# Attention with V scaled and the decay applied out of PSUM, routing in PSUM, and a new order inside the MoE step

## What is computed

```
# 1. attention with decay: B=4, H=8, S=768, head_dim=64
gamma[h] = 1 - 2 ** (-5 - h)
state = gamma * state + k_t v_t^T              # per head, 64 x 64
y_t   = q_t @ state / sqrt(64)
x = y as 3072 rows (tokens) of 512
# 2. mixture of experts: E=8, F=1024, one expert for each token
e = argmax(x @ w_gate)
x = softmax(x @ w_gate)[e] * sigmoid(x @ w_output_gate)[e] * (relu(x @ w1[e]) @ w2[e])
# 3. feed-forward: 512 -> 2048 -> 512
h = x @ w_in;  out = (h - tanh(h)) @ w_out
```

## Time and profile before

| | |
|---|---|
| time, median of 3 runs | 1131.85 us (1128.59 to 1132.87) |
| the profiled execution: time, span | 1125.78 us, 1124.0 us |
| granted TensorE clock over the span | 0.976 |
| busy: TensorE, VectorE, ACT, POOL | 1047.3, 784.1, 337.6, 382.6 us |
| attention | to about 157 us |
| MoE, with the tables ahead of it | about 157 to 559 us |
| feed-forward | about 559 us to the end |

### The profile page before, as it was taken

How to read it: one execution, slowest core, us unless ns; L and a number is a source line. 1 busy time by engine, 2 the same in 40 slices (tenths; PEclk the granted TensorE clock), 3 DMA queues, 4 the chain that set the end, 5 groups by cost and what they waited for, 6 DMA issues and landing times.

```text
span 1124.0 us, 18489 instructions
## 1 busy us (share of the span) xinstructions
PE 1047.3 (93%) x5577; PEld 866.1 (77%) x5578; DVE 784.1 (70%) x1267; ACT 337.6 (30%) x631; POOL 382.6 (34%) x316
## 2 busy tenths in 40 slices
PE   8988885999999979999679999999999999999998
PEld 7867684787777868878568887887888788788887
DVE  3888977555655556655257777877876877787775
ACT  2432322232322322222013333333333333333333
POOL 2455549665956786791470000000000000000000
PEclk9998998999999999999889999999999999999999
DMA  9976645767767677784320001001001000100101
GB/s 341 330 255 206 229 153 181 230 214 225 238 217 245 206 251 231 220 252 153 135 57 10 20 10 47 19 9 47 9 19 37 19 19 25 31 0 0 38 1 38
DMA packets 78308, 139.56 MB, mean 124 GB/s; under 512 B 7744, under 2 KB 39872, under 8 KB 78272
## 3 DMA queue, kind: packets, MB, share of 16 engines
q1 hardware_dynamic: 31280, 77.73, 21.0%
q10 hardware_dynamic: 43152, 48.77, 13.6%
q0 software_dynamic: 3840, 12.59, 3.4%
HBM read 100.00 MB, written 39.06 MB: 124 GB/s over the span
## 4 chain that ended last, share of the span: by engine, by line
PE 59%; DMA 17%; DVE 13%; issue 6%; ACT 2%; ACTq 1%; POOL 1%; DVEq 0%; SPq 0%; POOLq 0%
PE banks L1104 11%; PE banks L1106 10%; PE banks L1105 10%; DMA hid_quads<-hid_rows 7%; PE banks L1196 7%; PE banks L1198 7%; PE banks L1197 7%; DMA hid_rows<-hid 7%; DVE onehot L691 2%; DVE hidT L854 2%; DMA vn_sb<-in_vn 1%; PE banks L1005 1%; ACT hid L570 1%; PE banks L1012 1%; DVE q_scaled L713 1%
## 5 line engine op out<-in xcount | busy, mean ns | idle before, releaser
L397 POOL TENSOR_TENSOR w_sb<-raw,w_sb 128x1024 fp32r<-128x1024 f32 x80 | 198.3, 2479 | 6.7
L1196 PE MATMUL banks<-x2T_hi,w_sb 128*128 (+1 forms) x384 | 152.9, 398 | 5.2 <-DVE g_sb L947 5.2
L1198 PE MATMUL banks<-x2T_lo,w_sb 128*128 (+1 forms) x384 | 150.4, 392 | 0.0
L1197 PE MATMUL banks<-x2T_hi,w_sb 128*128 (+1 forms) x384 | 150.3, 391 | 0.0
L410 POOL DMA_INDIRECT gathered<-y_sorted,row_back x20 | 22.3, 1117 | 374.4 <-DVE x_sb L912 373.8
L1106 PE MATMUL banks<-w_sb,g_hi 128*128 128x512 f32 x384 | 149.4, 389 | 0.0
L1104 PE MATMUL banks<-w_sb,g_lo 128*128 128x512 f32 x384 | 149.4, 389 | 0.0
L1105 PE MATMUL banks<-w_sb,g_hi 128*128 128x512 f32 x384 | 149.4, 389 | 0.0
L854 DVE STREAM_TRANSPOSE hidT<-hid_quads 128x512 f32<-128x512 f32 x62 | 63.0, 1094 | 115.0 <-DMA hid_quads<-hid_rows 115.0
L1104 PE MATMUL banks<-w_sb,xsT_lo 128*128 (+1 forms) x248 | 101.5, 409 | 28.9 <-DVE xsT_lo L813 26.9
L622 ACT ACTIVATE square<-banks 128x512 f32<-128x512 f32 x96 | 57.4, 597 | 195.0 <-PE banks L1198 195.0
(11 more groups left out here) (135 smaller groups left out, 1890.7 us busy)
## 6 DMA issues: line engine op xcount, KB each, us to landing
raw<-in_weights SPq DMA_DIRECT2D x80, 512.0 KB, 4.0
hid_rows<-hid ACTq DMA_DIRECT2D x31, 512.0 KB, 4.1
hid_quads<-hid_rows ACTq DMA_DIRECT2D x31, 512.0 KB, 4.4
xs_sb<-x_sorted ACTq DMA_DIRECT2D x124, 64.0 KB, 3.0
y_sorted<-ys_sb ACTq DMA_DIRECT2D x31, 256.0 KB, 2.4
kT_sb<-in_kT SPq DMA_DIRECT2D x24, 256.0 KB
qT_sb<-in_qT SPq DMA_DIRECT2D x24, 256.0 KB
kn_sb<-in_kn SPq DMA_DIRECT2D x24, 256.0 KB
```

The source lines that it names most:

```text
L397: nc.gpsimd.tensor_tensor(w_sb[:, s, 1, lo:hi], raw[:, p % RAW_SLOTS], w_sb[:, s, 0, lo:hi].bitcast(fp32), ALU.subtract).then_inc(piece_do ...
L1196: T.matmul(out_, w_lo, hi, start=first, stop=False)
L1197: T.matmul(out_, w_hi, hi, start=False, stop=False)
L1198: return T.matmul(out_, w_hi, lo, start=False, stop=last)
```

## The change

Attention:

- V is scaled in place of K: POOL's `scale_values` multiplies V by the decay of its position, for all 24 tiles, and both `to_state` and `from_chunk` use the scaled V. The mask is then plain causal, one 128x128 table read by broadcast. Q isn't scaled at all: VectorE's `decay_rows` multiplies the sum in bank 3 by q_decay on its way to `xT_sb`. Only bank 3 is used for the sum, so `from_state` of the next tile waits for `decay_rows`.
- The tables of q_decay for chunks 1 to 5 are made by POOL (`make_q_decay`) from the first and a factor for each head; before, they were loaded. Inputs of a tile come in two transfers of 512 KB (keys and queries, then K and V by token). The tables and the zero fill of `x_sorted` are issued on ACT's queue.
- `rows_and_logits` takes the place of router parts, transposes and sum: four products of xT with the identity and the gates side by side, 144 columns each, into banks 5 and 6. ACT copies the rows out; VectorE's `add_logits` reduces over the four parts.
- `logits` and `ranked` lie in PSUM. The routing uses tensor_tensor with a broadcast operand in place of tensor_scalar and scalar_tensor_tensor. The ranks accumulate in one bank over the tiles, from the region's first row up, with an upper and a lower triangular product, so `seen` and the cast go. `find_row` has two instructions instead of four and runs two tiles behind.
- TensorE's order is from_chunk(c), rank(t - 2), scores(c + 1), from_state(c + 1), to_state(c + 1), rows_and_logits(t). `x_sb` has six slots instead of three. POOL waits for the first xsT_lo before it splits set 1.

MoE: a new order in the step, on ACT and on VectorE, and around the last tiles.

```diff
+            def scale_values(t):
...
+                nc.gpsimd.tensor_tensor(v_scaled[:, c % RING].rearrange("p (h d) -> p h d", h=HEADS),
+                                        vn_sb[:, c % RING].rearrange("p (h d) -> p h d", h=HEADS),
+                                        k_decay_sb[:, c].unsqueeze(2).to_broadcast([P, HEADS, HEAD_DIM]),
+                                        ALU.mult).then_inc(v_scaled_done, 1)
...
+            def add_logits(t, last=False):
...
+                V.reduce_sum(one(logits, t), x_parts[:, :, P:X_COLS].rearrange("p k e -> p e k"), AX).then_inc(logits_made, 1)
...
-                V.tensor_scalar(one(onehot, t), ranked[:, 0], route[:, 0:1], None, ALU.is_equal).then_inc(onehot_done, 1)
...
+                V.tensor_tensor(one(onehot, t), ranked[:, 1], route[:].to_broadcast([P, EXPERTS]), ALU.is_equal)\
+                 .then_inc(onehot_done, 1)
...
-                V.tensor_tensor(q_scaled[:, c % 2], qT_sb[:, c % RING], q_decay_sb[:, c], ALU.mult)\
-                 .then_inc(q_scaled_done, 1)
+            def decay_rows(t, c):
+                dve.wait_ge(y_done, t + 1)
+                V.tensor_tensor(xT_sb[:].rearrange("p a n -> p (a n)"), at(3), q_decay_sb[:, c], ALU.mult).then_inc(xT_made, 1)
...
+            def rows_and_logits(t, first=False):
+
+                pe.wait_ge(xT_made, t + 1)
+                if not first:
+                    pe.wait_ge(logits_made, t)
                 for k in range(DK):
-                    last = T.matmul(at(6)[k * GROUP:(k + 1) * GROUP, 0:P], gates_sb[:, k], xT_sb[:, k], start=True, stop=True)
...
+                    last = T.matmul(x_parts[:, k], xT_sb[:, k], ident_gates_sb[:, k], start=True, stop=True)
+                last.then_inc(x_done, 1)
...
+            pool.wait_ge(xsT_lo_done, 1)
             pool.wait_ge(tables_done, 1)
             split_pieces(0, 1)
```

The MoE step, ACT first and then VectorE:

```diff
                 relu(i, 0)
-                if number >= 1:
-                    hid_hi(i - 1, number - 1)
                 if number >= 3:
                     store_rows(i - 3)
                 relu(i, 1)
-                store_hidden(i)
+                store_hidden(i, number)
                 if number + 1 < MOE_TILES:
                     x_hi(i + 1)
+                if number >= 1:
+                    hid_hi(i - 1, number - 1)
                 load_hidden(i)
...
+            store_rows(MOE_TILES - 3)
             hid_hi(MOE_TILES - 1, MOE_TILES - 1)
-            for i in range(MOE_TILES - 3, MOE_TILES):
+            for i in (MOE_TILES - 2, MOE_TILES - 1):
                 store_rows(i)
...
                     copy_rows(i - 3)
+                if number + 1 < MOE_TILES:
+                    transpose_rows(i + 1)
                 if number >= 1:
                     transpose_hidden(i - 1)
                 if number + 1 < MOE_TILES:
-                    transpose_rows(i + 1)
+                    x_lo(i + 1)
                 if number >= 1:
                     hid_lo(i - 1, (number - 1) % 2)
-                if number + 1 < MOE_TILES:
-                    x_lo(i + 1)
...
             last = MOE_TILES - 1
+            dve.wait_ge(ys_stored, 16 * (last - 2))
+            copy_rows(last - 2)
             transpose_hidden(last)
             hid_lo(last, last % 2)
-            for i in range(last - 2, last + 1):
+            for i in (last - 1, last):
                 dve.wait_ge(ys_stored, 16 * i)
                 copy_rows(i)
```

More of the change, by code:

```diff
@@ L323, in _ @@
                 sp.sem_inc(out_stored[m], 16)
[L324 to L335, removed]
-                attention_inputs(0, c)
[L337 to L343, removed]
+            for c in range(CHUNKS):
+                attention_inputs(0, c)
             for t in range(CHUNKS, TOKEN_TILES):
@@ new lines, in _ @@
+            pool.wait_ge(k_decay_ready, 16)
+            scale_values(0)
+            pool.wait_ge(q_decay_ready, 32)
+            make_q_decay(1)
+            scale_values(1)
+            make_q_decay(2)
+            scale_values(2)
+            for c in range(3, CHUNKS):
+                make_q_decay(c)
+            for t in range(TOKEN_TILES):
+                if t + RING < TOKEN_TILES:
+                    scale_values(t + RING)
+                if t == 2:
+                    pool.wait_ge(heads_zeroed, 16)
+                if t >= 2:
+                    scatter(t - 2)
@@ new lines, in _ @@
+            act.dma_start(causal_sb[:], causal).then_inc(mask_ready, 16)
+            act.dma_start(k_decay_sb[:], k_decay).then_inc(k_decay_ready, 16)
+            act.dma_start(q_decay_sb[:, 0], q_decay).then_inc(q_decay_ready, 16)
+            act.dma_start(q_step_sb[:], q_step).then_inc(q_decay_ready, 16)
+            for dst, src in ((ident_gates_sb, ident_gates), (small_sb, small), (ident, small[:, small.shape[1] - P:])):
+                act.dma_start(dst[:], src).then_inc(tables_loaded, 16)
@@ L747, in _ @@
             sequence(BATCH - 1, last=True)
-            choose_expert(TOKEN_TILES - 1, (TOKEN_TILES - 1) % 2)
-            find_row(TOKEN_TILES - 1)
+            last_t = TOKEN_TILES - 1
+            find_row(last_t - 1)
+            add_logits(last_t, last=True)
+            choose_expert(last_t)
+            find_row(last_t)
             links = [0]
@@ L1023, in from_chunk @@
                         rows = slice(half * HEAD_DIM, (half + 1) * HEAD_DIM)
-                        last = T.matmul(at(3 + c % 2)[rows, pair * P:(pair + 1) * P], vn_sb[:, c % RING, cols],
+                        last = T.matmul(at(3)[rows, pair * P:(pair + 1) * P], v_scaled[:, c % RING, cols],
                                         probs[:, half * PAIRS + pair], start=c == 0 and pair == 0, stop=True,
@@ L1092, in _ @@
             sequence(BATCH - 1, last=True)
-            last_t = TOKEN_TILES - 1
-            stay_warm(WARM_TAIL[1], still)
-            rank(last_t, last_t % 2)
-            pe.wait_ge(seen_done, 3 + TOKEN_TILES)
-            pe.wait_ge(x_copied, TOKEN_TILES)
-            T.matmul(at(5)[:, 0:EXPERTS], ones_bf[:], seen[:, 0], start=True, stop=True).then_inc(counts_done, 1)
+            rank(TOKEN_TILES - 2)
+            stay_warm(WARM_TAIL[1], still, 0)
+            rank(TOKEN_TILES - 1)
+            count_chunk(TOKEN_TILES - 1, True)
             def split_product(out_, hi, lo, w_hi, w_lo, first, last):
@@ L1239, in decay_tables @@
     s = np.arange(P)
[L1240 to L1242 removed]
+    causal = s[None, :] >= s[:, None]
     token = np.arange(SEQ).reshape(CHUNKS, P)
```

319 lines of the change are left out of this document (156 added, 163 removed).

## The result

The changed kernel takes 1078.44 us (median of 4, 1074.69 to 1083.84) against 1130.22 for the kernel before (median of 4, 1126.03 to 1132.87): a ratio of 0.9549 [0.9492, 0.9605]. Its profiled execution took 1083.84 us, the longest of its four, with a span of 1082.1; that of before, 1125.78, was shorter than each of its four. A difference of the two spans alone gives 41.9 us.

What follows compares the result with a forecast made beforehand. TensorE, busy 93% of the span, was taken to bound the kernel. Attention and its edges 21.5, MoE 12.6 and its end 9.5 sum to 43.6 us off the median of 1131.85: 1088 us, range 1080 to 1106.

Steps and rivals of the forecast that it cites:

- (c): Attention: the routing is not freed from POOL, or input DMA paces the stage; 20 us back, 1108; chance 0.06.
- (a): Attention: VectorE paces it, its dependent instructions with gaps needing 5.8 us an interval and not 4.6; 1098; chance 0.15.
- intervals: Attention, from_chunk(0) to from_chunk(23): 23 intervals fall from 143.0 to 123.6 us, at 5.38 each with 2 for input stalls.
- start: Start of attention: keys and queries load first, so from_chunk(0) starts at 10.2 us instead of 12.44; -2.2.
- End of attention: Behind from_chunk(23): routing and find_row calls come before the last row is written, one subtraction more for counts; +0.8 us.
- First xsT_lo: Start of MoE: POOL waits for it, so it takes 0.68 us instead of 1.40 beside POOL; -0.7.
- MoE, -12.6: MoE step: x_hi and x_lo ahead of the hidden tile's work leave 3 of TensorE's 15.6 us of waits.
- its end, -9.5: Last MoE tiles: copying first cuts the gap before rows_out(29) by 7.3 us; the slow clock after it gives 2.2.
- (b): MoE: the gaps stay because row loads set them; 12.6 us back, 1100; chance 0.15.
- (d): MoE: slower than before, as the new order closes a loop through row-load landings; 1140 at landings of 7.0; chance 0.03.
- 6.1 under the median: Whole kernel: the profiled execution, 1125.78 us, lay 6.1 under the median of 1131.85; the saving was taken off the median.
- The rule against the row: Attention routing: the skill's 62 extra cycles per PSUM source mean about 0.45 us more an interval; the profile row means nothing.

Runs made afterwards that it cites:

- e5: The changed kernel with `logits` and `ranked` put back from PSUM into SBUF, all else as changed: 1092.06 us, ratio 0.9658.
- e11: The changed kernel with the one-hot row made by tensor_scalar again, its input still in PSUM: 1080.23 us, ratio 0.9575.
- e10b: The kernel before with one edit, `ranked` placed in a free part of PSUM bank 7 instead of SBUF: 1110.68 us, ratio 0.9828.
- e3: The kernel before, attention untouched, with all of the new order of the MoE step and its last tiles: 1104.9 us, ratio 0.9793.
- e4: The kernel before with only the last MoE tiles changed (rows copied and stored earlier): 1119.9 us, ratio 0.9918.
- e12: The kernel before with POOL's splits of the first eight pieces, and the loads of the last four, moved behind attention: 1118.48 us, one execution.
- e7: The changed kernel with POOL waiting for the second xsT_lo instead of the first before splitting set 1: 1075.96 us, ratio 0.9503.
- e1: The changed kernel unchanged, timed in more rounds beside the kernel before: 1078.96 us, ratio 0.9562.
- e6: The changed kernel with the MoE row loads issued ahead of the hidden tile's work: 1072.76 us, ratio 0.9484.

## Why the prediction was right in kind and short in size

**The mechanism of attention: right, but put too widely.** VectorE instructions with all inputs in SBUF were held behind POOL and those with an input in PSUM were not; e5, e11 and e10b show it from both sides. "SBUF alone" is not enough to be held, though: reductions with one SBUF input (L689 and L853 above) never were. Rival (c) is out, and so is (a): VectorE is busy 60% of the stretch.

**The term "intervals", -19.4: mis-sized, it is about -25.** Two parts. The first is where it started from: 143.0 us of one profiled execution. e3 and e4, with that same attention, have 148.6 and 145.9, so the mean is 145.8. The second is where it ends: 119.7 to 121.5 instead of 123.6. The interval is 5.21 and not 5.38 (`to_state` takes 0.90, 92.44 to 93.34, where 0.99 was put, and `rows_and_logits` 1.07 where 1.11 was), and the 2 us for input stalls never came: from 10 to 131 us TensorE waits only for `add_logits`, 3.6 us in seven places, and for no transfer. Nor did I weigh the edits against each other: moving `ranked` to PSUM gives 18 of the 27 by itself (e10b).

**The term "start", -2.2: right at 10.14 and wrong as a gain.** The forecast of 10.2 was met to 0.1. But 12.44 was particular to one execution: the old start is at 10.08, 11.19, 10.63 and 10.89 in e3, e4, e10b and e12, 11.05 with the 12.44 in the mean. Of the nine profiles with the new attention, e11 has 11.84 and the other eight 9.19 to 10.25. The gain is about 0.9.

**End of attention, +0.8: too careful**, nothing was measured (5.8 and 5.8). **First xsT_lo, -0.7:** 1.40 became 0.69, as put, and xsT_lo(1) starts 28.6 us behind `from_chunk(23)` instead of 29.8. POOL's splits hold the tables between the two as they did before the change (L846 takes 2.22 us, its like L834 took 2.26), so that is time that the change left where it was. The prediction checked POOL's lateness for TensorE alone, not whom POOL holds; e7 starts xsT_lo(1) 5.3 us earlier.

**MoE, -12.6, and its end, -9.5: right in sum, with the waits mis-sized.** The two are 22.1; the stage has 373.4, 376.1, 379.4 and 380.2 us with the old order and 349.2 to 355.9 with the new one, means of 377.3 and 353.1 (e3, after, e1, e5, e7, e11): 24. Split at the end of the third last `rows_out`, 8.8 of these are the end and 15 the part ahead of it. Yet TensorE's waits from the third tile on fell from 15.6 to 6.3, by 9.3 and not 12.6: I kept 3 us of waits and twice that stayed. What else the stage won isn't shown. The row load was the next to be late, as said, since e6 takes these waits away. Two of my signs failed. TensorE was to wait at most 4 us for xsT_lo and waited 6.3. VectorE's waits for xs_sb came to 121 us where 25 was to make the forecast wrong; that one counted idle time of an engine that has slack, and e6 shows what it was worth. Rivals (b) and (d) are out.

**"6.1 under the median": the step behind both sizes.** I took 43.6 from a profile of before and put its 6.1 on the result, as if they lay where nothing changes. They lay in the stages that the change shortens: the profile of before is the shortest of its kind in the intervals and in MoE. With the means over all profiles, start and intervals give 26, xsT_lo(1) 1 and MoE 24, less 1 to 1.5 us that the feed-forward half is longer: 50, and 50.7 to 51.8 were measured. Against the one profile, the forecast looks better than it was: 43.6 were summed and the spans differ by 41.9. That is luck. The intervals fell by 22.6 there instead of 19.4 and the MoE stage by 17.5 instead of 22.1, and the profile of after is the longest of its four.

**The rule against the row.** By the Trainium skill (VectorE: DVE Perf Modes, the errata section) the routing would take 62 cycles more an instruction from PSUM, an estimated 65 ns at the 0.96 GHz of that page. The same instructions take 166, 166 and 174 ns in the kernel after and 161, 161 and 167 in e5 (L706, L699, L704): 5 to 7 ns. The row decides, and rival (a) had no footing.

## What to carry to other kernels

A small VectorE instruction that ends when something on POOL ends is being held; put one of its inputs in PSUM, or POOL's work elsewhere, and look which instruction is next in line for the hold, since clearing one may free two. Before sizing a gain from a stall, read the stall in several executions: here it varied by 5.6 us in one stage while the stage freed of it varied by 1.8. Where two in-order queues feed each other, change both orders together: ACT's half of this one alone cost 30 us (VectorE's alone wasn't tried).

## What was unexpected of the hardware

A hold depends on a tenth of a microsecond. With q_scaled 0.15 us behind POOL's subtraction it took 2.75 us; with it 0.13 ahead, 0.68, and POOL paid 0.4. What set VectorE back in the kernel before stands in its timeline just ahead of the earlier trace rows:

```profile
95.35 1.01 POOL L417 DMA_INDIRECT x_sorted<-x_sb,row_at  x1 [3.85 <-DVE row_at L704]
...
95.90 2.73 DVE L691 TENSOR_SCALAR onehot<-ranked,route 128x8 f32 x1 [0.16 <-DVE route L689]
96.39 1.05 POOL L430 TENSOR_TENSOR k_scaled<-kn_sb,k_decay_sb 128x512 f32<-128x512 f32 x1
...
97.55 1.05 POOL L393 TENSOR_SCALAR w_sb<-raw 128x1024 fp32r<-128x1024 f32 x1
98.67 0.16 DVE L693 TENSOR_TENSOR seen<-seen,onehot 128x8 bf16<-128x8 bf16 x1
```

The one-hot row starts 0.55 us into POOL's scatter and is held across the end of it, k_scaled and the split's first half, to 98.63; by then q_scaled meets the second half from behind. So a hold can last over several POOL instructions that follow one another closely, though the VectorE instruction was there before all but the first. In e12, without the split, such a row ends with k_scaled, after 1.58 us (91.91), and where no k_scaled follows it ends with the scatter, after 0.43 (97.07). A scatter doesn't hold all that is beside it: near the end of attention in the kernel before a row that starts 0.28 us into one takes 0.23 (159.86). By which rule the pair changes hands wasn't measured. And VectorE's `seen`, 8 numbers of bf16, was held for 1610 ns as soon as it was first in line, where it had taken 258 in the kernel before.
